# First expert layer: the subtraction that makes the next weights' low parts goes from GpSimd to VectorE, and the picks, prefix sums and places move into the middle of a tile

## The chip, the core and the metric

The kernel runs on one core of a Trainium2 chip. The metric is the device time of one execution in microseconds (us). Before the change it was 1570.85 us, the median of 3 runs (1567.33 to 1571.03).

## The reference

Three stages follow each other on 9984 rows of 256 numbers: a squared-ReLU attention without softmax over 4 batches of 2496 rows, then two mixture-of-experts layers with 8 experts each, hidden width 1024. The first layer only treats rows whose skip score is positive and adds its result to the row; the second treats all rows, with a bias on the gate by modality, and replaces the row.

```python
scores = (1.0 / S) * z @ z.T;  x = u * (relu(scores) ** 2 @ v)
# layer 1, for rows with x @ w_skip > 0
e = argmax(x @ w_gate);  g = softmax(x @ w_gate)[e]
x = x + g * (relu(x @ w1[e]) @ w2[e])
# layer 2, for all rows
logits = x @ w_gate2 + modality_bias[modality_id]
e = argmax(logits);  g = softmax(logits)[e]
out = g * (relu(x @ w1b[e]) @ w2b[e])
```

## The kernel before, in words

All products are made in single precision from two parts: a value is split into a rounded high part and a low part (value minus high), and three matmuls (high x high, high x low, low x high) are summed in PSUM.

The attention stage writes every row, with its gate and logits, to a table in device memory (`token_rows`), sorted by expert. Each expert layer (`ph` 0, then 1) is a loop over the experts, and inside it a hardware loop over tiles of 256 rows (`for t in lo..hi`, bounds read from the device's own counts). Every engine has its own instruction stream with the same loops, and semaphores join them; nothing but the order of the text sets the order within an engine. `t == lo` is the first tile of an expert.

One tile on TensorE (PE): `layer1(p)` for p = 0 to 3 makes the hidden columns (12 matmuls each, into pO), `layer2(p)` multiplies them with w2 (12 matmuls each, into pS), in the order layer1(0), layer1(1), the transposes of the next tile's rows (L1378), layer1(2), layer2(0), layer1(3), layer2(1), layer2(2), layer2(3). `layer2(p)` waits for VectorE's low part of hidden quarter p (`h_low(p)`, L1159), which waits for ScalarE's high part (`h_high(p)`, L785), which waits for layer1(p). `layer2(0)` also waits until VectorE has read the last tile's result out of pS (`y_out`; the instructions L1179 to L1186, called "the y group" below).

In the first layer a tile's result rows need routing for the second layer, one tile later: `pick_expert` on VectorE (L1109 to L1118: argmax and one-hot), `exp_tile` on ScalarE (L755), `prefix_x2` on PE (L1403 to L1405: how many rows stand ahead of each), `stage_rows` on ScalarE (L751: copy of the rows for the scatter; it waits until the last scatter has landed), `place_tile` on VectorE (L1130 to L1140: destination of each row), and two indirect DMAs from GpSimd (POOL; L579: the scatter).

The next expert's weights are in `raw` while an expert is at work. ScalarE casts them to the high parts in 4 pieces of 1024 columns (`split_high`, L633), spread over the first tile of an expert. POOL subtracts them for the low parts (`split_low`, L466, 8 instructions of 512 columns), then issues the load of the weights after those (L453, L454: 2 MB). POOL also loads w2 transposed (L458), from which PE makes gate columns at the start of an expert (L1360).

Between the layers VectorE routes the last tile, counts (`finish_groups`, up to L1073) and only then can PE enter the second layer; PE fills that time with matmuls that keep it warm (L1214).

Of the kernel before, what the change touches and what calls it, by code (L numbers as in the profile page):

```python
# [5 lines left out]
F32 = mybir.dt.float32  # L6
# [4 lines left out]
ALU = mybir.AluOpType  # L11
# [7 lines left out]
E, F = 8, 1024  # L19
# [20 lines left out]
WP = 4  # L40
# [15 lines left out]
def bass_attention_two_moe(nc, u, v, z, w_skip, w_gate, w1, w2, modality, w_gate2, bias2, w2t, out):  # L56
    xs = nc.dram_tensor("token_rows", (GR * CAP + SPARE, ROW), F32, kind="Internal").ap()

    with ExitStack() as ctx:
# [359 lines left out]
        def _(pool):  # L419
# [59 lines left out]
            def next_weights(turn_, slot):  # L479

                split_low(turn_ + 1, 1 - slot)
                e = pool.value_load(order[0:1, turn_ + 2:turn_ + 3], min_val=0, max_val=2 * E - 1)
                wait(wl_ready, WP * turn_ + 2 * WP)
                load_weights(e)
# [65 lines left out]
            for ph in range(2):  # L550
# [6 lines left out]
                for at in range(E):  # L557
# [3 lines left out]
                    def ahead():  # L561
                        if ph == 0:
                            if at + 2 < E:
                                wait(gcols_made, at + 2)
                                load_w2t(at + 2)
                            next_weights(turn_, at % 2)
                        else:
                            with pool.If(hi < total):
                                next_weights(turn_, at % 2)

                    with pool.If(lo < hi):
                        with pool.Fori(lo, hi) as t:
                            with pool.If(t == lo):
                                ahead()
# [6 lines left out]
                            else:  # L581
# [15 lines left out]
        def _(act):  # L597
# [130 lines left out]
            for ph in range(2):  # L728
# [31 lines left out]
                for at in range(E):  # L760
# [19 lines left out]
                    with act.If(lo < hi):  # L780
                        with act.Fori(lo, hi) as t:
                            def h_high(p):
                                act.wait_ge(q.h_psum, 4 * t + p + 1)
                                act.wait_ge(q.h_used, 4 * t + p + 1)
                                s_.activation(hH[p], pO[:, p * 512:(p + 1) * 512], ACT.Relu).then_inc(q.h_hi, 1)  # L785
                            def start(piece):
                                with act.If(t == lo):
                                    ahead((piece,))

                            h_high(0)  # L790
                            start(0)
                            h_high(1)
                            take_x(t + 1, (t + 1) % 2)
                            h_high(2)
                            keep_x(t + 1, (t + 1) % 2)
                            start(1)
                            if ph == 0:
                                with act.If(t > 0):
                                    exp_tile(t)
                            h_high(3)  # L800
                            start(2)
                            if ph == 0:
                                with act.If(t > 0):
                                    stage_rows(t)
                            start(3)
# [13 lines left out]
        def _(dve):  # L819
# [265 lines left out]
            for ph in range(2):  # L1085
# [55 lines left out]

                xt_low(0, 0)
# [4 lines left out]
                for at in range(E):  # L1147
                    hi = end_of(dve, ph, at)
                    if ph == 0:
# [5 lines left out]
                    with dve.If(lo < hi):  # L1155
                        with dve.Fori(lo, hi) as t:
# [4 lines left out]
                            h_low(0)  # L1161
                            h_low(1)
                            xt_low(t + 1, (t + 1) % 2)
                            h_low(2)
                            if ph == 0:
                                with dve.If(t > 0):
                                    pick_expert(t)
                            h_low(3)
                            par = t % 2
# [20 lines left out]
                            if ph == 0:  # L1190
                                with dve.If(t > 0):
                                    place_tile(t)
# [10 lines left out]
        def _(pe):  # L1203
# [186 lines left out]
            for ph in range(2):  # L1390
# [17 lines left out]
                for at in range(E):  # L1408
# [6 lines left out]
                    with pe.If(lo < hi):  # L1415
                        pe.wait_ge(wl_ready, WP * (at + 1 + ph * E))
                        pe.sem_inc(pe_passed, 1)
                        with pe.Fori(lo, hi) as t:
# [41 lines left out]
                            layer2(0)  # L1460
                            layer1(3)
# [3 lines left out]
                            last_tile(prefix_x2)  # L1465
# [33 lines left out]
```

## Time and profile before

| | |
|---|---|
| median of 3 runs | 1570.85 us |
| profiled execution | 1574.07 us, span 1572.3 us |
| PE busy | 1514.6 us (96%) |
| VectorE (DVE) busy | 1013.3 us (64%) |
| ScalarE (ACT) busy | 776.4 us (49%) |
| POOL busy | 466.1 us (30%) |
| mean granted TensorE clock | 0.988 |

Times in the rows are from the span's start. The attention stage fills about the first 740 us, the first expert layer about 750 to 1068 us, the second about 1083 to 1570 us. A PE that is busy 96% of the span still leaves some 58 us idle, and where those lie is what the rows further down show. A row's bracket gives the idle time of that engine just before the instruction, and who ended it.

### The profile page before, as it was taken

How to read it: one execution, taken by the hardware profiler on the slowest of the kernel's cores; microseconds unless marked ns; L12 is line 12 of the kernel's file. 1: busy time of each engine (PE TensorE's matmuls, PEld its weight loads, DVE VectorE, ACT ScalarE, POOL GpSimd, SP SyncE). 2: the span in 40 equal slices, each digit the busy share in tenths (PEclk: the TensorE clock that was granted, in tenths of full speed). 3: DMA queues.
4: the chain of work that ended last, by engine and by line, in shares of the span. 5: the costliest groups of instructions: out<-in, count | busy, mean ns of one | idle time of the engine just before them, and what ended most of it. 6: DMA issues, size and time to landing. Idle time of an engine off the chain costs nothing.

```text
span 1572.3 us, 38375 instructions
## 1 busy us (share of the span) xinstructions
PE 1514.6 (96%) x13409; PEld 1379.5 (88%) x13409; DVE 1013.3 (64%) x2382; ACT 776.4 (49%) x1463; POOL 466.1 (30%) x434
## 2 busy tenths in 40 slices
PE   8999999999999999998999999998999999999996
PEld 6878887788778887887988988988999999999996
DVE  7989977888788989876566666654333333333332
ACT  6677766676677767663444434443322322322321
POOL 4133412343133324222444444443211111111111
PEclk9999999999999999999999999998999999999998
DMA  5311031203002022112433333321311111111110
GB/s 114 95 42 49 27 109 33 63 31 99 27 29 62 27 82 80 30 40 92 139 126 114 127 129 126 99 79 46 101 48 41 48 54 41 48 48 41 48 48 26
DMA packets 60108, 106.41 MB, mean 68 GB/s; under 512 B 18183, under 2 KB 32018, under 8 KB 59980
## 3 DMA queue, kind: packets, MB, share of 16 engines
q1 hardware_dynamic: 41788, 46.66, 10.8%
q0 software_dynamic: 18192, 58.13, 10.8%
q8 instruction: 70, 1.15, 0.3%
q14 instruction: 58, 0.48, 0.1%
HBM read 75.35 MB, written 30.94 MB: 68 GB/s over the span
## 4 chain that ended last, share of the span: by engine, by line
PE 78%; DMA 6%; DVE 4%; issue 4%; POOL 3%; ACT 2%; POOLq 0%; DVEq 0%; SPq 0%; ACTq 0%
PE pO L1238 29%; PE pO L1430 18%; PE pS L1446 18%; PE pS L1227 8%; DMA token_rows<-xrow,dest 4%; POOL VL L466 2%; DMA raw<-in_v_dram 2%; PE pT L1378 1%; PE pT L1286 1%; DVE take L1110 1%; DMA A<-in_w2t_dram 1%; PE pO L1247 1%; DVE take L1109 1%; PE pM L1296 1%; PE pO L1360 1%
## 5 line engine op out<-in xcount | busy, mean ns | idle before, releaser
L1430 PE MATMUL pO<-ZH,VH 128*128 x2016 | 402.5, 288 | 2.3 <-issue 2.3
L1446 PE MATMUL pS<-VL,AH 128*128 128x256 f32 (+1 forms) x2016 | 370.3, 284 | 21.5 <-DVE AL L1159 21.5
L785 ACT ACTIVATE AH<-pO 128x512 fp32r<-128x512 f32 x252 | 151.0, 599 | 401.7 <-PE pO L1430 401.4
L1446 PEld LDWEIGHTS pS<-VL,AH 128*128 128x128 f32 x2016 | 311.8, 190 | 25.3 <-DVE AL L1159 25.2
L1430 PEld LDWEIGHTS pO<-ZH,VH 128*128 128x128 f32 x2016 | 328.3, 192 | 4.0 <-issue 4.0
L961 DVE TENSOR_TENSOR AL<-A,AH 128x512 fp32r<-128x512 f32 (+1 forms) x400 | 305.1, 763 | 13.7
L1238 PE MATMUL pO<-AH,VH 64*128 64x512 f32 (+1 forms) x1520 | 301.0, 386 | 3.7 <-DVE xT L870 2.3
L1238 PE MATMUL pO<-AH,VL 64*128 64x512 f32 (+1 forms) x1520 | 298.7, 383 | 0.0
L1238 PE MATMUL pO<-AL,VH 64*128 64x512 f32 (+1 forms) x1520 | 298.3, 382 | 0.0
L1159 DVE SCALAR_TENSOR_TENSOR AL<-pO,AH 128x512 fp32r<-128x512 f32 x252 | 172.7, 691 | 187.9 <-ACT AH L785 184.1
L659 ACT ACTIVATE R<-pS 128x512 f32<-128x512 f32 (+1 forms) x400 | 213.6, 587 | 157.5 <-PE pS L1227 148.4
L1430 PE MATMUL pO<-ZL,VH 128*128 x1008 | 286.0, 284 | 0.0
L1446 PE MATMUL pS<-VL,AL 128*128 128x256 f32 (+1 forms) x1008 | 284.6, 282 | 0.0
L959 DVE CAST AH<-A 128x512 fp32r<-128x512 f32 (+1 forms) x400 | 231.2, 578 | 44.6 <-ACT A L668 43.3
L668 ACT ACTIVATE A<-R 128x512 f32<-128x512 f32 (+1 forms) x400 | 228.1, 624 | 9.5 <-DVE AL L961 9.5
L1430 PEld LDWEIGHTS pO<-ZL,VH 128*128 128x128 f32 x1008 | 193.9, 192 | 0.0
L584 POOL DMA_INDIRECT out_dram<-xrow,tok_at x80 | 77.8, 973 | 382.9 <-DVE tok_at L1188 370.4
L1446 PEld LDWEIGHTS pS<-VL,AL 128*128 128x128 f32 x1008 | 190.8, 189 | 0.0
L1238 PEld LDWEIGHTS pO<-AH,VH 64*128 64x128 f32 x1520 | 147.8, 185 | 28.4 <-issue 3.4
L1238 PEld LDWEIGHTS pO<-AL,VH 64*128 64x128 f32 x1520 | 148.0, 185 | 23.2
L1238 PEld LDWEIGHTS pO<-AH,VL 64*128 64x128 f32 x1520 | 147.8, 185 | 22.3
L515 POOL TENSOR_TENSOR xT<-xT,uT 128x512 f32<-128x512 f32 x38 | 50.7, 1344 | 294.7 <-DVE xT L870 294.7
(194 smaller groups left out, 1584.4 us busy)
## 6 DMA issues: line engine op xcount, KB each, us to landing
raw<-in_w_dram POOLq DMA_DIRECT2D x22, 1024.0 KB, 7.1
xin<-token_rows SPq DMA_DIRECT2D x65, 268.0 KB
uT<-in_u_dram SPq DMA_DIRECT2D x16, 512.0 KB
A<-in_w2t_dram POOLq DMA_DIRECT2D x8, 1024.0 KB
raw<-in_v_dram SPq DMA_DIRECT2D x4, 1152.0 KB, 5.9
raw<-in_v_dram SPq DMA_DIRECT2D x4, 768.0 KB, 7.6
raw<-in_z_dram SPq DMA_DIRECT2D x8, 368.0 KB
token_rows<-pad_row SPq DMA_DIRECT2D x10, 268.0 KB
```

The costliest lines, as they stand in the source:

```text
L515: g_.tensor_tensor(xT[:, d, :], xT[:, d, :], uT[:, d, :], ALU.mult).then_inc(x_ready, 1)
L584: g_.indirect_dma_start(out, bass.IndirectOffsetOnAxis(tok_at[:, s_:s_ + 1], 0), x2a[:, s_, 0:D], None, bounds_check=N - 1, oob_is_err=Fal ...
L659: s_.activation(R[k % 2][:, 0:n], pS[k % 2][:, 0:n], ACT.Relu, scale=1.0 / S).then_inc(relu_done, 1)
L668: s_.activation(A[k % NA][:, 0:n], R[k % 2][:, 0:n], ACT.Square).then_inc(square_done, 1)
L785: s_.activation(hH[p], pO[:, p * 512:(p + 1) * 512], ACT.Relu).then_inc(q.h_hi, 1)
L959: v_.tensor_copy(AH[k % NBUF][:, 0:n], A[k % NA][:, 0:n]).then_inc(ah_ready, 1)
L961: v_.tensor_tensor(AL[k % NBUF][:, 0:n], A[k % NA][:, 0:n], AH[k % NBUF][:, 0:n].bitcast(F32), ALU.subtract).then_inc(al_ready, 1)
L1159: v_.scalar_tensor_tensor(out=hL[p], in0=pO[:, p * 512:(p + 1) * 512], scalar=0.0, in1=hH[p].bitcast(F32), op0=ALU.max, op1=ALU.subtract). ...
L1227: last = t_.matmul(pS[r][:, 0:n], w[rows, (2 * p + r) * P:(2 * p + r + 1) * P], x[rows, zc:zc + n], start=(m == 0), stop=(m == 2))
L1238: last = t_.matmul(pO[:, (KD * r + d) * QW:(KD * r + d) * QW + n], vv[rows, vo + k * D + d * P:vo + k * D + (d + 1) * P], a[k % NBUF][rows ...
L1430: last = t_.matmul(pO[:, p * 512 + fi * TT:p * 512 + (fi + 1) * TT], w[h][:, kd, f * P:(f + 1) * P], x[:, ds(par, 1), kd, :].rearrange("p ...
L1446: last = t_.matmul(pS[s][:, 0:width], a[p][:, fi * TT + s * P:fi * TT + (s + 1) * P], w[h][:, f, 0:width], start=(f == 0 and n == 0), stop ...
```

## The change

In the first layer only:

- VectorE makes the low parts of the next weights: `next_low`, 4 instructions of 1024 columns after `h_low(3)` of an expert's first tile, ahead of the y group. POOL makes none there any more. In the second layer and in the attention stage POOL still does.
- `pick_expert` moves from behind `h_low(2)` to behind `h_low(0)`; `place_tile` from behind the y group to behind `h_low(2)`.
- On PE the prefix sums move from the end of the tile to behind `layer2(0)`.
- On POOL the scatter of a tile stands ahead of the weight loads.

In both layers ScalarE's 4 casts stand together behind `h_high(3)`; in the first, `exp_tile` and `stage_rows` now stand around `h_high(2)`, ahead of `keep_x`, the copy of the next tile's rows.

```diff
-            def next_weights(turn_, slot):
-                split_low(turn_ + 1, 1 - slot)
+            def next_weights(turn_, slot, split):
+                if split:
+                    split_low(turn_ + 1, 1 - slot)
...
-                            with pool.If(t == lo):
-                                ahead()
                             if ph == 0:
                                 with pool.If(t > 0):
                                     wait(q.dest, t)
...
+                            with pool.If(t == lo):
+                                ahead()
...
                             h_high(0)
-                            start(0)
                             h_high(1)
                             take_x(t + 1, (t + 1) % 2)
-                            h_high(2)
-                            keep_x(t + 1, (t + 1) % 2)
-                            start(1)
                             if ph == 0:
                                 with act.If(t > 0):
                                     exp_tile(t)
+                                    h_high(2)
+                                    stage_rows(t)
...
+                            keep_x(t + 1, (t + 1) % 2)
                             h_high(3)
-                            start(2)
...
+                            with act.If(t == lo):
+                                ahead(range(WP))
...
+                def next_low(turn_, slot):
+                    for n, (raw, wh, wl) in enumerate(weight_pieces(slot)):
+                        dve.wait_ge(wh_ready, WP * turn_ + n + 1)
+                        v_.tensor_tensor(wl, raw, wh.bitcast(F32), ALU.subtract).then_inc(wl_ready, 1)
...
                             h_low(0)
+                            if ph == 0:
+                                with dve.If(t > 0):
+                                    pick_expert(t)
                             h_low(1)
                             xt_low(t + 1, (t + 1) % 2)
                             h_low(2)
                             if ph == 0:
                                 with dve.If(t > 0):
-                                    pick_expert(t)
+                                    place_tile(t)
                             h_low(3)
+                            if ph == 0:
+                                with dve.If(t == lo):
+                                    next_low(turn_ + 1, 1 - at % 2)
...
-                            if ph == 0:
-                                with dve.If(t > 0):
-                                    place_tile(t)
...
                             layer2(0)
+                            last_tile(prefix_x2)
                             layer1(3)
                             layer2(1)
                             layer2(2)
                             layer2(3)
-                            last_tile(prefix_x2)
```

VectorE before, in a tile of the first layer, from the end of the pick on: `AL<-pO,AH` is `h_low(3)`, and `xrow<-pS,xkeep` opens the y group.

```order
L1118 TENSOR_TENSOR oh<-eq,take 128x2x8
L1166 UNCONDITIONAL_BRANCH
L1158 REGISTER_ALU
L1159 SCALAR_TENSOR_TENSOR AL<-pO,AH 128x512
L1170 REGISTER_ALU
L1179 ISA
L1179 REGISTER_ALU
L1179 SCALAR_TENSOR_TENSOR xrow<-pS,xkeep 128x256
```

VectorE now, at the same place: `dest<-dest_f,take` ends the place, and the two rows at L1143 are the four subtractions, run only where `t == lo`.

```order
L1137 TENSOR_TENSOR dest<-dest_f,take 128x2
L1173 UNCONDITIONAL_BRANCH
L1162 REGISTER_ALU
L1163 SCALAR_TENSOR_TENSOR AL<-pO,AH 128x512
L1177 COMPARE_AND_BRANCH
L1143 TENSOR_TENSOR VH<-raw,VH 128x1024 x2
L1143 TENSOR_TENSOR VL<-raw,VL 128x4x256 x2
L1177 UNCONDITIONAL_BRANCH
L1180 REGISTER_ALU
L1189 ISA
L1189 REGISTER_ALU
L1189 SCALAR_TENSOR_TENSOR xrow<-pS,xkeep 128x256
```

So between `h_low(3)` and the y group there are now four subtractions, and the place has gone from behind the y group to a point ahead of `h_low(3)`.

ScalarE before, from `h_high(2)` on: `xkeep<-xin` is `keep_x`, the casts from `raw` stand one by one.

```order
L785 ACTIVATE AH<-pO 128x512
L739 ISA
L739 COPY xkeep<-xin 128x536
L787 COMPARE_AND_BRANCH
L633 CAST VH<-raw 128x1024
L787 UNCONDITIONAL_BRANCH
L798 COMPARE_AND_BRANCH
L755 ACTIVATE ex<-lsh 128x2x8
L798 UNCONDITIONAL_BRANCH
L783 REGISTER_ALU
L785 ACTIVATE AH<-pO 128x512
```

ScalarE now, from `h_high(2)` on, with `stage_rows` (`xrow<-xrow`) between it and `keep_x`.

```order
L786 ACTIVATE AH<-pO 128x512
L751 ISA
L752 COPY xrow<-xrow 128x536
L791 UNCONDITIONAL_BRANCH
L784 REGISTER_ALU
L786 ACTIVATE AH<-pO 128x512
L795 UNCONDITIONAL_BRANCH
L740 ISA
L740 COPY xkeep<-xin 128x536
L784 REGISTER_ALU
L786 ACTIVATE AH<-pO 128x512
```

The copy for the scatter has come ahead of the last quarter's high part, and no cast stands between the quarters any more.

## Rows read from the trace of the kernel before

**Rows 1.** Stages: engines' busy us (x instructions), granted clock, DMA share, GB/s.

```profile
750.00:1069.00 319.00, 297.49 (x2585) 290.24 (x2585) 196.07 (x610) 131.34 (x235) 140.61 (x128) 0.99 0.35 115
1069.00:1084.00 15.00, 9.34 (x103) 8.88 (x101) 7.74 (x44) 1.88 (x4) 3.88 (x4) 0.75 0.14 46
1084.00:1572.00 488.00, 474.42 (x3999) 474.21 (x3998) 176.45 (x360) 143.34 (x244) 89.64 (x90) 0.99 0.16 49
```

**Rows 2.** PE's wait between 750 and 1069 us: us, times, longest.

```profile
PE pS L1446 <- DVE AL L1159: 21.5, 18, 2.7
```

**Rows 3.** Timeline of PE: start, us; transposes of four tiles.

```profile
765.46 0.38 PE L1378 MATMUL pT<-ident,xin 128*128 128x128 f32 x2
...
777.63 0.27 PE L1378 MATMUL pT<-ident,xin 128*128 128x128 f32 x1
...
791.17 0.38 PE L1378 MATMUL pT<-ident,xin 128*128 128x128 f32 x2
...
1057.26 0.38 PE L1378 MATMUL pT<-ident,xin 128*128 128x128 f32 x2
```

**Rows 4.** Timeline of the third expert's three tiles, 829 to 871 us.

```profile
835.90 5.04 POOL L466 TENSOR_TENSOR VH<-raw,VH 128x512 fp32r<-128x512 f32 x4
...
837.28 3.70 DVE L1110 TENSOR_SCALAR take<-take 128x2 f32<-128x2 f32 x1
...
850.31 0.51 PE L1446 MATMUL pS<-VL,AH 128*128 128x264 f32 x2 [0.69 <-DVE AL L1159]
...
852.44 1.02 POOL L579 DMA_INDIRECT token_rows<-xrow,dest  x1 [0.30 <-issue]
...
859.36 0.64 ACT L751 COPY xrow<-xrow 128x536 f32<-128x536 f32 x1 [4.88 <-DMA token_rows<-xrow,dest]
...
863.80 0.39 PE L1446 MATMUL pS<-VL,AH 128*128 128x264 f32 x1 [0.99 <-DVE AL L1159]
```

**Rows 5.** Stages again: a stretch with a lower granted clock.

```profile
910.00:920.00 10.00, 7.29 (x49) 6.97 (x49) 6.77 (x16) 3.16 (x5) 8.08 (x8) 0.83 0.42 150
```

**Rows 6.** Timeline of an undisturbed tile of the first layer.

```profile
768.78 0.16 DVE L1109 TENSOR_SCALAR take<-xrow 128x2 f32<-128x2 f32 x1
...
770.30 0.17 DVE L1118 TENSOR_TENSOR oh<-eq,take 128x16 bf16<-128x16 f32 x1
...
770.41 0.60 ACT L785 ACTIVATE AH<-pO 128x512 fp32r<-128x512 f32 x1 [0.60 <-PE pO L1430]
...
775.06 0.49 DVE L1179 SCALAR_TENSOR_TENSOR xrow<-pS,xkeep 128x256 f32<-128x256 f32 x1 [3.33 <-PE pS L1446]
...
776.12 0.17 DVE L1186 COPY xrow<-xkeep 128x6 f32 x1
...
779.50 0.41 PE L1446 MATMUL pS<-VL,AH 128*128 128x264 f32 x2
```

**Rows 7.** VectorE's subtraction in the attention stage (ns), and one beside a scatter.

```profile
L961 DVE TENSOR_TENSOR AL<-A,AH x400: 624/693/1709, 10.7 to 725.0; 128x512 fp32r<-128x512 f32 x107, 128x448 fp32r<-128x448 f32 x27
...
674.31 0.74 DVE L961 TENSOR_TENSOR AL<-A,AH 128x512 fp32r<-128x512 f32 x1
674.32 0.97 POOL L496 DMA_INDIRECT token_rows<-xrow,dest  x1 [0.30 <-issue]
```

**Rows 8.** POOL's weight loads, and ScalarE's cast.

```profile
L633 ACT CAST VH<-raw 128x1024 fp32r<-128x1024 f32 x16 | 16.8, 1048 | 0.0
...
849.88 0.92 POOL L454 DMA_DIRECT2D raw<-in_w_dram  x1
```

**Rows 9.** Timeline between the two layers.

```profile
1075.10 6.01 PE L1214 MATMUL pS<-ones 128*128 128x128 bf16 x64
1077.59 0.64 ACT L751 COPY xrow<-xrow 128x536 f32<-128x536 f32 x1 [4.70 <-DMA token_rows<-xrow,dest]
...
1081.75 0.17 DVE L1073 CAST pad_from<-base_t 128x8 int32<-128x8 f32 x1
...
1083.39 0.57 PE L1430 MATMUL pO<-ZH,VH 128*128 x1 [2.28 <-issue]
```

More of the change, by code:

```diff
@@ L565, in ahead @@
                                 load_w2t(at + 2)
-                            next_weights(turn_, at % 2)
+                            next_weights(turn_, at % 2, False)
                         else:
                             with pool.If(hi < total):
-                                next_weights(turn_, at % 2)
+                                next_weights(turn_, at % 2, True)
                     with pool.If(lo < hi):
                         with pool.Fori(lo, hi) as t:
-                            with pool.If(t == lo):
-                                ahead()
                             if ph == 0:
@@ L580, in _ @@
                                                               bounds_check=GR * CAP - 1, oob_is_err=False).then_inc(q.stored, 16)
-                            else:
+                            with pool.If(t == lo):
+                                ahead()
+                            if ph == 1:
                                 wait(q.y2_out, t + 1)
@@ L785, in h_high @@
                                 s_.activation(hH[p], pO[:, p * 512:(p + 1) * 512], ACT.Relu).then_inc(q.h_hi, 1)
-                            def start(piece):
-                                with act.If(t == lo):
-                                    ahead((piece,))
                             h_high(0)
-                            start(0)
                             h_high(1)
                             take_x(t + 1, (t + 1) % 2)
-                            h_high(2)
-                            keep_x(t + 1, (t + 1) % 2)
-                            start(1)
                             if ph == 0:
@@ L799, in _ @@
                                     exp_tile(t)
-                            h_high(3)
-                            start(2)
-                            if ph == 0:
-                                with act.If(t > 0):
-                                    stage_rows(t)
-                            start(3)
+                                    h_high(2)
+                                    stage_rows(t)
+                                with act.Else():
+                                    h_high(2)
+                            else:
+                                h_high(2)
+                            keep_x(t + 1, (t + 1) % 2)
+                            h_high(3)
+                            with act.If(t == lo):
+                                ahead(range(WP))
                     with act.Else():
@@ L1148, in _ @@
                     hi = end_of(dve, ph, at)
+                    turn_ = at + ph * E
                     if ph == 0:
@@ L1189, in _ @@
                                 v_.memset(mx[:, 0:1, 0:1], 0.0).then_inc(q.y_out, 1)
-                            if ph == 0:
-                                with dve.If(t > 0):
-                                    place_tile(t)
+                    if ph == 0:
+                        with dve.Else():
+                            next_low(turn_ + 1, 1 - at % 2)
                     lo = hi
```

## The prediction, made before the changed kernel was run

> **What bounds the kernel now.** I read the stages first, then the waits of the one that the change touches, then its timeline. In the stages [rows 1] the reader sees that PE is busy 297.5 of 319 us in the first expert layer, 9.3 of 15 us between the layers, and 474 of 488 us in the second layer. So what PE waits for is what can be won, and it lies mostly in the first layer. In its waits [rows 2] one pair holds PE: layer2 waits for VectorE's low part of a hidden quarter, 18 times, 21.5 us. VectorE itself is idle a third of that stage (196 of 319 us busy), so it isn't out of throughput; it is late at certain places.
>
> How much that costs in all is read from the distance of the tiles [rows 3]. Two undisturbed tiles are 777.63 - 765.46 = 12.17 us apart; with a change of expert between them (gate columns) it is 791.17 - 777.63 = 13.54 us. From 765.46 to the last tile at 1057.26 there are 21 steps, 7 of them changes of expert: 14 x 12.17 + 7 x 13.54 = 265.2 us, and the trace takes 291.8. That is 26.6 us too much, and with the wait of about 1.5 us in the last tile, which lies behind 1057.26, 28 us. 21.5 of them are the waits; 2 x 1.7 are two drops of the granted clock from 2.4 to 1.2 GHz, of which the rows show one [rows 5] (10 x 0.17), both beside long waits of PE (it is busy only 7.3 of 10 us there); the rest hides in the modelled ends of the matmuls.
>
> The timeline of one expert [rows 4] shows three causes. (a) In the first tile a two-column TENSOR_SCALAR of the pick takes 3.70 us: it starts at 837.28 and ends at 840.98, within 0.04 us of the end of POOL's four subtractions (835.90 + 5.04). Undisturbed, the same group runs from 768.78 to 770.47 as a whole [rows 6]. `h_low(3)` stands behind it, and so does layer2. (b) In the second tile the y group and the place stand ahead of `h_low(0)`: PE waits 0.69 us. (c) POOL, held up by subtractions and loads, issues its scatter at 852.44 only, ScalarE's `stage_rows` waits 4.88 us for it to land, the y group waits for that copy, and `h_low(0)` is late again: 0.99 us.
>
> **The change part by part.** POOL's 8 subtractions per expert go, and with them (a) whole: nothing else of POOL's runs long enough to hold VectorE for 3 us. The scatter now goes ahead of the loads, so (c) goes: a scatter that is issued in mid tile has about a tile, 12.17 us, until `stage_rows` of the next tile asks for it, and even behind weight loads it needed 859.36 - 852.44 = 6.9 us. The place leaves the stretch between the y group and `h_low(0)`, and (b) goes: without it `h_low(0)` can start when ScalarE has the high part. All of the 28 us is therefore open.
>
> Here a rule of the Trainium skill bears on (a). SBUF — State Buffer, section "Who interferes with whom", says that whoever issues first gets the port pair that VectorE and GpSimd share for its whole instruction. By it the small instruction would wait for the end of one GpSimd instruction, 5.04 / 4 = 1.26 us, where the trace shows 3.70 us, the end of the run of four. By the rule removing (a) would be worth less than half of what it is by the row; the sum goes by the row.
>
> What is added is 4 subtractions of 1024 columns on VectorE. The trace has none of that width. From below: 693 ns for 512 columns, 624 ns for 448 [rows 7], so 69 ns for 64 columns and 0.69 + 8 x 0.069 = 1.25 us for 1024. From above: twice 0.69 = 1.39 us undisturbed, and twice 1.71 = 3.4 us if each ran at the longest that this instruction ever took. I take 1.25: a single instruction has its fixed part once. ScalarE's casts at 1.05 us [rows 8] are faster and don't pace it.
>
> Where it lies, counted from `h_high(3)` of an expert's first tile as zero (770.41 in the clean tile [rows 6]): the first cast is ready at 0.5 + 1.05 = 1.6, the subtractions end at 1.6 + 4 x 1.25 = 6.6. The y group, so far at 775.06 (4.65), comes at 6.6 + 0.35 (register steps) and takes 776.12 + 0.17 - 775.06 = 1.23: it ends at 8.15, and `h_low(0)` at 8.85. PE asks for it at 779.50, which is 9.1. So it is hidden with 0.25 us to spare. A group of 12 matmuls takes (9.09 - 0.5) / 6 = 1.43 us, since six of them and the transposes (0.5 us) lie in those 9.09 us. Behind `h_low(0)` the pick takes 1.6 us beyond its start, to about 10.4, and PE's prefix sums now ask for it at 9.1 + 1.43 = 10.5; the place (1.5 us), `h_low(1)` to `h_low(3)` and the next rows' low part (0.6 us from one start to the next) take 1.5 + 4 x 0.6 more, to about 14.4, where layer2(3) asks at 10.6 + 3 x 1.43 = 14.9. Every step fits with little to spare, in the tile behind the first one of each expert. The cover is thin, and one thing eats it: the y group ends with a small copy, and the pick begins with small TENSOR_SCALARs, just when POOL issues the two weight loads (0.76 and 0.92 us [rows 8]), and rows show that such instructions can be held by POOL. Bounds for the new wait: 0 and 1.68 - 0.25 = 1.4 us per expert. I take 0.6, for 8 experts 5 us (0 to 11).
>
> The new waits on one engine: on ScalarE `exp_tile` stands ahead of `h_high(2)`, and behind it queue `h_high(2)`, `stage_rows`, `keep_x` and `h_high(3)`. The pick's part that it waits for ends 0.8 us after `h_low(0)`, at 9.6 in the worst tile, when layer1(2) has only just ended (9.1); layer2(2) asks at 13.5. Nothing. The later `keep_x` delays the load of the next rows by about 2 us of a slack that no wait in [rows 2] has ever used. The load of w2 transposed comes some 7 us later in the expert and is wanted at the next one's start, over 12 us on; every expert here has 2 or 3 tiles. In the second layer ScalarE's casts stand in one block of 4.2 us behind `h_high(3)`, and the next `h_high(0)` comes four groups of PE, 5.7 us, after it: hidden. I cost these at nothing.
>
> Between the layers [rows 9]: `stage_rows` of the last tile waits 4.70 us for a scatter that was issued late, because the place stood behind the y group; and the whole routing of the last tile hangs on it, up to the counts at 1081.75, and PE enters at 1083.39. With the place in mid tile that scatter has landed, and the pick comes about 1.2 us earlier: the counts come 5.5 us earlier, at 1076.2. But PE's 64 warming matmuls take 6.01 us and end at 1081.1 today. They start when the prefix sums have ended, 1.2 us earlier, so they end at 1079.9 and PE can enter 1.5 us later: at 1081.4. The granted clock of this stretch is 0.75 on average [rows 1]; at the full clock throughout they would take some 2 us less, and PE would enter at about 1079.2. So the gain is 2.0 to 4.2 us, with 0 and 5.5 as outer bounds; I take 3.
>
> Sum: -28 + 5 - 3 = -26 us. The profiled execution, 1574.07 us (span 1572.3, 1.8 us around it), would be 1548; it lies 3.2 us above the median of the runs, so on that scale 1570.85 - 26 = 1544.8 us.
>
> **The rivals.** First, the gain is halved by a wait that takes the place of the removed one: the four subtractions meet POOL's scatter of the same tile. For it speaks the narrow cover above: every us on them is a us on PE. If each of the two scatter DMAs (0.97 us) held them, the y group would come 1.9 us later, less 0.25, and with the same again in part for the prefix sums some 2 us per expert: 8 x 2 = 16 instead of 5 us, 1570.85 - 28 + 16 - 3 = 1556 us. Against it: in the attention stage the same instruction met a scatter alone 57 times, the first at 93.34 us and the last at 674.31, and took 0.69 to 0.76 us [rows 7]. The skill's same section speaks for it: a VectorE instruction with two SBUF inputs contends with a GpSimd instruction that reads SBUF, as the scatter reads its indices; by that rule the 57 should have been held, and the trace does not agree.
>
> Second, slower than before: VectorE becomes the bound of the tile behind each expert's first. Its place is the four subtractions, its price their length. They cost PE nothing up to 1.25 us, and the gain of 31 us is used up when each takes 1.25 + (31 / 8 + 0.25) / 4 = 2.3 us. At 3.4 us, the upper bound, the loss would be 8 x (4 x 2.15 - 0.25) = 67 us and the time 1570.85 - 31 + 67 = 1607 us. For it: this instruction did take 1.71 us at 512 columns. Against it: that was beside subtractions or products of POOL, and in the first layer POOL has none of these left.
>
> Third, no change: PE's waits only move, because the real limit of the late tiles is the landing of the scatter, and that is no faster. It would have to be over 12 us on the way; 6.9 us is the most seen here. 1571 us.
>
> **How the numbers follow.** The forecast, with its own range of 1538 (28 + 4.2 won, nothing lost) to 1552, has 0.67; the halved gain 0.21; slower 0.06; no change 0.03; a gain above all bounds, by the clock, 0.03. The predicted time is the forecast's, 1544.8 us. The range goes from 1538 to 1558 and leaves out the last three cases and the tail of the second. A difference of 0.3% (4.7 us) is about what a measurement of this kernel can tell from no change. Faster: 0.67 + 0.21 + 0.03 = 0.91; within 0.3%: 0.03; slower: 0.06.
>
> **What would show it.** Right: the small instructions of the pick all at 0.2 to 0.5 us; no wait of `stage_rows` for the scatter; four subtractions near 1.25 us per expert; tiles 12.2 us apart within an expert; PE's waits for `h_low` under 6 us in the layer; the second layer 11.8 us per tile as before; PE entering it right behind the warming matmuls. Wrong: subtractions over 2 us; PE waiting for the one-hot or for `h_low(0)` in every second tile by over 1 us; waits of PE for rows or weights that it never had; a second layer whose tiles have grown.

## The result, and the profile after

The changed kernel took 1543.69 us (median of 4 runs, 1540.86 to 1543.97) beside 1570.18 us for the kernel before on the same chip: 0.983 of the time, 95% interval 0.981 to 0.985. Measured again on another occasion (run 9 below) it was 1544.12 us and 0.983 (0.982 to 0.985). The prediction said 1544.8. The number was right, and, as the rows below show, partly because errors of opposite sign met.

The stages of the profiled execution (1540.86 us, span 1539.2), columns as in [rows 1]:

```profile
750.00:1045.00 295.00, 293.19 (x2667) 289.40 (x2665) 201.19 (x683) 130.65 (x238) 70.28 (x68) 1.00 0.38 125
...
1054.00:1539.00 485.00, 467.00 (x3932) 466.59 (x3930) 173.28 (x356) 139.80 (x239) 89.67 (x90) 0.98 0.16 48
```

In the first layer PE is now busy all but 1.8 us. Its waits from 744 to 1100 us, all but one of 0.7 and one of 0.5 us, as in [rows 2]:

```profile
PE pS L1456 <- DVE AL L1163: 3.2, 1, 3.2
PE pO L1380 <- DVE pad_from L1070: 2.9, 1, 2.9
PE pM L1413 <- DVE oh L1115: 1.6, 1, 1.6
...
```

The 18 waits for low parts (21.5 us) are gone. The one that is left, 3.2 us, isn't in the first layer at all: it ends at 1077.50, in the third tile of the second. The transposes of PE, the answer to [rows 3]:

```profile
762.71 0.60 PE L1388 MATMUL pT<-ident,xin 128*128 128x128 f32 x4
774.89 0.60 PE L1388 MATMUL pT<-ident,xin 128*128 128x128 f32 x4
788.48 0.60 PE L1388 MATMUL pT<-ident,xin 128*128 128x128 f32 x4
1027.06 0.60 PE L1388 MATMUL pT<-ident,xin 128*128 128x128 f32 x4
```

12.18 us from tile to tile and 13.59 with a change of expert; the 21 steps take 1027.06 - 762.71 = 264.35 us, where they took 291.8 and an undisturbed run of them was put at 265.2. (That was about 1 us too high: at the last change of expert there are no gate columns to make, and that step takes at most 12.4 us.)

The VectorE subtractions, and the small TENSOR_SCALAR that was held for 3.70 us in [rows 4] (ns, minimum, median, maximum). "Held" means here: much longer than the same instruction is undisturbed, and at its end together with an instruction of GpSimd.

```profile
L1143 DVE TENSOR_TENSOR VH<-raw,VH x16: 1219/1222/1226, 757.2 to 1010.5; 128x1024 fp32r<-128x1024 f32 x16
```
```profile
L1107 DVE TENSOR_SCALAR take<-take x23: 168/169/657, 763.7 to 1038.8; 128x2 f32<-128x2 f32 x23
```

One turn of the weights in the third expert, with the tile behind it, in which everything was to fit narrowly:

```profile
831.53 0.60 ACT L786 ACTIVATE AH<-pO 128x512 fp32r<-128x512 f32 x1 [1.39 <-PE pO L1440]
...
833.10 2.36 DVE L1143 TENSOR_TENSOR VH<-raw,VH 128x1024 fp32r<-128x1024 f32 x2 [0.24 <-ACT VH L634]
...
833.46 1.70 POOL L578 DMA_INDIRECT token_rows<-xrow,dest  x1 [0.30 <-issue]
...
835.38 2.36 DVE L1143 TENSOR_TENSOR VL<-raw,VL 128x1024 fp32r<-128x1024 f32 x2
...
838.70 0.16 DVE L1196 COPY xrow<-xkeep 128x6 f32 x1
838.77 0.68 DVE L1163 SCALAR_TENSOR_TENSOR AL<-pO,AH 128x512 fp32r<-128x512 f32 x1
...
839.23 0.91 POOL L454 DMA_DIRECT2D raw<-in_w_dram  x1
...
839.56 0.57 DVE L1107 TENSOR_SCALAR take<-take 128x2 f32<-128x2 f32 x1
...
840.45 0.41 PE L1456 MATMUL pS<-VL,AH 128*128 128x264 f32 x2
...
841.29 0.17 DVE L1115 TENSOR_TENSOR oh<-eq,take 128x16 bf16<-128x16 f32 x1
...
841.90 0.18 PE L1413 MATMUL pM<-oh,before 128*128 128x16 bf16 x1
```

Counted from `h_high(3)` at 831.53, rounded: the subtractions end at 6.2 (predicted 6.6), the y group at 7.3 (8.15), `h_low(0)` at 7.9 (8.85), PE asks at 8.9 (9.1); the one-hot is there at 9.9 (10.4) and asked for at 10.4 (10.5). The cover, the time from a value being ready to PE asking for it, is 1.0 us and 0.4 us, where 0.25 and 0.1 were predicted. The 0.57 us of the TENSOR_SCALAR, 0.17 undisturbed, lie beside a weight load of GpSimd (839.23 + 0.91 = 840.14, the TENSOR_SCALAR ends at 840.13); 0.66 is the longest of it.

Between the layers, the answer to [rows 9]:

```profile
1040.37 0.18 PE L1413 MATMUL pM<-oh,before 128*128 128x16 bf16 x1 [1.60 <-DVE oh L1115]
...
1041.19 3.74 PE L1224 MATMUL pS<-ones 128*128 128x128 bf16 x64
...
1045.63 0.38 PE L1440 MATMUL pO<-ZH,VH 128*128 x1 [0.71 <-DVE ZL L1093]
```

The 64 warming matmuls take 3.74 us instead of 6.01: the granted clock was 1.00 from 1041.2 to 1045.6, where it was 0.60 from 1075.1 to 1081.1 before. What differs just ahead of them is PE's wait for the one-hot between the layers, 1.60 us now and 3.07 before; behind the 3.07 us the clock had fallen to 0.50. Waits further back don't explain it: run 4 below has waits of up to 5.4 us in its first layer and 1.39 here, and its warming takes 3.74 us; run 3 has hardly any in the first layer and 3.3 us here, and takes 4.59. Run 7 doesn't fit so simply, with 1.61 us here and 5.36 us of warming; its first layer has eight waits of 1.2 us. What decides there stays open.

The start of the second layer is new:

```profile
1060.28 5.07 POOL L466 TENSOR_TENSOR VL<-raw,VL 128x512 fp32r<-128x512 f32 x4
...
1066.13 0.77 POOL L453 DMA_DIRECT2D raw<-in_w_dram  x1 [0.78 <-POOL VL L466]
...
1069.48 1.02 POOL L585 DMA_INDIRECT out_dram<-xrow,tok_at  x1 [0.30 <-issue]
...
1075.90 0.88 DVE L1194 TENSOR_SCALAR xrow<-pS,xkeep 128x256 f32<-128x256 f32 x2 [9.21 <-DMA out_dram<-xrow,tok_at]
...
1076.76 0.68 DVE L1163 SCALAR_TENSOR_TENSOR AL<-pO,AH 128x512 fp32r<-128x512 f32 x1
...
1077.50 0.80 PE L1456 MATMUL pS<-VL,AH 128*128 128x256 f32 x2 [3.20 <-DVE AL L1163]
```
```profile
1060.43 0.60 PE L1388 MATMUL pT<-ident,xin 128*128 128x128 f32 x4
...
1072.27 0.60 PE L1388 MATMUL pT<-ident,xin 128*128 128x128 f32 x4
...
1088.83 0.60 PE L1388 MATMUL pT<-ident,xin 128*128 128x128 f32 x4
```
```profile
1070.00:1074.00 4.00, 4.00 (x36) 4.00 (x35) 0.00 (x0) 1.75 (x3) 0.51 (x1) 1.00 1.03 339
1074.00:1078.00 4.00, 0.80 (x5) 0.60 (x4) 2.10 (x7) 1.24 (x2) 0.26 (x1) 0.87 0.23 84
1078.00:1082.00 4.00, 4.00 (x27) 4.00 (x27) 1.24 (x3) 0.07 (x1) 1.68 (x2) 0.70 0.46 134
```

Read the first block from the bottom: PE waits in the third tile for `h_low(0)`, which stands on VectorE behind the second tile's y group; that waits until the first tile's result rows have left their buffer. The DMA that takes them is issued at 1069.48, behind the subtractions and both weight loads, and 2 MB of weights fill the DMA engines ahead of it (share 1.03, 339 GB/s). VectorE goes on 6.4 us after its issue. PE's wait is 3.2 us, and the clock falls behind it. The two stretches behind 1074 lose 4 x 0.13 + 4 x 0.30 = 1.7 us by it, of which 3.2 x 0.08 = 0.3 us lie in the wait itself (granted clock 0.92 from 1074.3 to 1077.5) and cost nothing: about 1.5 us more. The tile steps say the same: 11.84 us from transposes to transposes, and 16.56 here, 4.7 more. It happens once, since the second layer has a single set of subtractions and weight loads, in its first tile.

So by stage, in the two profiles: from the first expert's gate columns (746.36 before, 744.35 after) to the first warming matmul (1068.20 and 1036.36; 40 of them stand ahead of the 64 above) 321.8 us before and 292.0 after (-29.8); from there to the first matmul of the second layer 15.2 and 9.3 (-5.9); the second layer 488.9 and 493.6 (+4.7). What lies ahead of the first layer differs by 2.0 us with no edit in it; over all the profiled executions, before and below, it varied from 742.9 to 746.4.

### The profile page after: what moved, and what is told of

It reads as the page before. It is cut to its first block, busy times and chain, and to the rows that moved or that the text cites. A ratio compares the mean times of both kernels' runs of the same rounds, so it can differ in the third digit from the quotient of the medians.

```text
span 1539.2 us, 38120 instructions
## 1 busy us (share of the span) xinstructions
PE 1501.9 (98%) x13409; PEld 1369.7 (89%) x13409; DVE 1010.4 (66%) x2414; ACT 773.9 (50%) x1463; POOL 391.2 (25%) x370
## 3 DMA queue, kind: packets, MB, share of 16 engines
q8 instruction: 70, 1.15, 0.3%
## 4 chain that ended last, share of the span: by engine, by line
PE 91%; DMA 3%; issue 2%; POOL 1%; DVE 1%; ACT 1%; SPq 0%; DVEq 0%; POOLq 0%; ACTq 0%
PE pO L1248 31%; PE pO L1440 23%; PE pS L1456 23%; PE pS L1237 9%; PE pT L1388 2%; DMA raw<-in_v_dram 2%; PE pT L1296 1%; DMA A<-in_w2t_dram 1%; PE pO L1257 1%; PE pM L1306 1%; PE pO L1370 1%; POOL VL L504 0%; DMA out_dram<-xrow,tok_at 0%; ACT R L660 0%; POOL VL L466 0%
```

## The experiments

Ten runs, in the order in which they were taken. "Layer 1", "between" and "layer 2" are the three stretches just named. The kernel before was run beside each, median 1569.5 to 1570.2 us. Runs 1, 2, 9 and 10 are medians of 5 executions, 5 and 8 of 10, the others of 4.

| run | what | median us | ratio, 95% | layer 1 | between | layer 2 |
|---|---|---|---|---|---|---|
| | before | 1570.2 | 1 | 321.8 | 15.2 | 488.9 |
| | changed | 1543.7 | 0.983 (0.981 to 0.985) | 292.0 | 9.3 | 493.6 |
| 1 | casts spread in layer 2 | 1537.5 | 0.979 (0.977 to 0.981) | 292.9 | 9.3 | 489.8 |
| 2 | rows written first in layer 2 | 1537.3 | 0.980 (0.978 to 0.982) | 291.9 | 9.3 | 489.8 |
| 3 | subtraction alone | 1543.7 | 0.984 (0.981 to 0.986) | 295.0 | 13.5 | 490.0 |
| 4 | moves alone | 1588.6 | 1.012 (1.010 to 1.014) | 339.9 | 9.1 | 492.0 |
| 5 | before, GpSimd pieces halved | 1577.8 | 1.004 (1.002 to 1.006) | 328.5 | 15.0 | 490.6 |
| 6 | one subtraction more | 1548.5 | 0.986 (0.984 to 0.988) | 298.3 | 9.3 | 493.4 |
| 7 | two more | 1558.8 | 0.992 (0.990 to 0.994) | 307.3 | 10.6 | 494.1 |
| 8 | before, one-element TENSOR_SCALARs | 1567.1 | 0.998 (0.997 to 0.999) | 320.1 | 13.3 | 487.4 |
| 9 | changed, again | 1544.1 | 0.983 (0.982 to 0.985) | 292.0 | 9.3 | 494.1 |
| 10 | edits of 1 and 2 | 1537.7 | 0.979 (0.978 to 0.980) | 292.5 | 9.3 | 489.7 |

**Runs 1, 2, 9 and 10: the second layer.** Run 1 gives the second layer its spread casts back, on ScalarE:

```diff
                             h_high(0)
+                            start(0)          # ph == 1, t == lo: ahead((0,))
...
                             keep_x(t + 1, (t + 1) % 2)
+                            start(1)
                             h_high(3)
-                            with act.If(t == lo):
-                                ahead(range(WP))
+                            if ph == 0:
+                                with act.If(t == lo):
+                                    ahead(range(WP))
+                            start(2)
+                            start(3)
```

> The changed kernel, with ScalarE's four casts of the second layer at their old places in the tile (behind the first, third and fourth quarter), the first layer untouched. The changed kernel's trace has one wait of 3.20 us of PE in the second layer and a drop of the granted clock behind it, in the tile after the first; before there was none. Theory: the casts in one block behind the fourth quarter start POOL's subtractions some 6 us later, these and the weight loads hold up POOL's scatter of the finished rows, the tile's result group on VectorE waits for the scatter's landing, and layer2(0) with it. Then this kernel has no such wait and takes 3.2 + 1.7 = about 5 us less than the changed one, some 1539 us. Rival: the wait comes from something else that the second layer inherited (the earlier entry, the load of rows), then it stays and the time is 1544 us.

Run 2 moves the loads on GpSimd instead, and leaves the casts in a block:

```diff
-                            with pool.If(t == lo):
-                                ahead()
+                            if ph == 0:
+                                with pool.If(t == lo):
+                                    ahead()
                             if ph == 1:
                                 wait(q.y2_out, t + 1)
...
+                                with pool.If(t == lo):
+                                    ahead()
```

> The changed kernel, with POOL's scatter ahead of the subtractions and weight loads in the second layer too, as the change does it in the first; the casts stay in one block. Theory: it is the scatter's place behind the subtractions that makes VectorE's result group wait in the second tile; with the scatter first the wait of 3.20 us goes and the time is about 1539 us, as with the casts spread. Rival: the subtractions themselves hold VectorE in that tile wherever the scatter stands; then PE still waits 2 to 4 us for a low part and the time stays at 1544 us.

Both took the wait away, and 6 us. (PE's wait lies in the layer's third tile, one later than run 1's expectation says.) In run 2 the rows leave before the subtractions:

```profile
1060.31 0.97 POOL L586 DMA_INDIRECT out_dram<-xrow,tok_at  x1 [15.39 <-DVE tok_at L1201]
...
1062.58 5.06 POOL L466 TENSOR_TENSOR VH<-raw,VH 128x512 fp32r<-128x512 f32 x4
```

In run 1 GpSimd subtracts early instead, and its weight loads, and the rows behind them, come sooner: 15.7 us after the layer's first matmul (1047.16) and not 20.5 (1066.13 - 1045.63):

```profile
1062.85 0.77 POOL L453 DMA_DIRECT2D raw<-in_w_dram  x1 [0.78 <-POOL VL L466]
```

VectorE still sits idle until the rows have landed in both runs, 4.9 and 5.0 us, as in the kernel before (5.0); in the changed kernel it was 9.2 us, and only that reached PE.

Runs 9 and 10 put the changed kernel and both edits together side by side.

> The changed kernel as it is, five rounds, beside the next run. Theory (the second layer's first tile costs it 4 to 5 us, and runs 1 and 2 each took that away): 1543 to 1544 us again, and over 4 us more than the next run. Rival (the 6 us between the changed kernel and runs 1 and 2 lay in the chip or in the hour, since they were measured on another occasion): 1537 to 1540 us, level with the next run.

> The changed kernel with both edits of runs 1 and 2: in the second layer the casts are spread over the first tile as in the kernel before, and GpSimd writes a tile's result rows before it subtracts and loads. Theory (each edit alone removes the same wait): 1537 us, as each alone, since there is nothing left for the second edit to remove; no wait of TensorE for VectorE in the second layer. Rival (each removed a part of it): 1534 to 1535 us.

1544.12 (1541.92 to 1544.86) against 1537.70 us (1536.54 to 1538.77): the ranges and the intervals are apart, so the 6 us are the kernel's and not the occasion's, and the second edit has nothing left to remove. In run 9's profile the wait is there again, 3.4 us. By the profiles the second layer is 3.8 to 4.4 us shorter; the other 2 us lie in executions that were not profiled (the profiled one was the changed kernel's fastest both times), and stay open. Each of the kernels of runs 1, 2 and 10 beats both the changed one and the one before.

**Run 3: the subtraction alone.** The four subtractions stay on VectorE; picks, prefix sums, places, scatter, casts and `stage_rows` go back to where they were.

```diff
+                            h_high(2)
+                            keep_x(t + 1, (t + 1) % 2)
+                            start(1)
...
                             h_low(0)
-                            if ph == 0:
-                                with dve.If(t > 0):
-                                    pick_expert(t)
                             h_low(1)
...
-                                    place_tile(t)
+                                    pick_expert(t)
...
+                                with dve.If(t > 0):
+                                    place_tile(t)
```

> The kernel before with only the subtraction moved: VectorE makes the four low parts of the first layer behind the fourth quarter of an expert's first tile; picks, prefix sums, places, casts and scatters stay where they were. Theory: the hold of 3.7 us goes (PE 1.8 us per expert), but the place still stands between the result group and the next first quarter and now begins some 2 us later, so PE waits 1 to 2 us there, and the scatter still lands late. Net 1 us per expert: about 1561 us, a third of the gain. Rival: POOL's subtractions were the whole cause, so this alone brings the time to about 1545 us.

The rival was right: layer 1 falls from 321.8 to 295.0 us, 27 of the 30 us, with every move undone. Its waits of PE, and ScalarE's wait for the late scatter:

```profile
PE pM L1417 <- DVE oh L1119: 3.3, 1, 3.3
...
PE pS L1460 <- DVE AL L1167: 1.4, 4, 0.6
```
```profile
ACT xrow L752 <- DMA token_rows<-xrow,dest: 31.0, 10, 4.5
```

The one-hot's wait of 3.3 us lies between the layers. `stage_rows` still waits ten times, 31 us, and PE loses 1.4 us by it at most. The moves are worth 3.0 us in layer 1 and 4.2 between the layers, and their casts in a block lose 3.6 in layer 2; the medians, 1543.71 and 1543.69, show nothing of the difference.

**Run 4: the moves alone.** All moves stay; GpSimd subtracts.

```diff
-                            next_weights(turn_, at % 2, False)
+                            next_weights(turn_, at % 2, True)
...
-                            if ph == 0:
-                                with dve.If(t == lo):
-                                    next_low(turn_ + 1, 1 - at % 2)
```

> The changed kernel with the subtraction of the first layer back on POOL: picks, prefix sums, places, the block of casts and the scatter ahead of the loads as in the changed kernel. Theory: the casts in one block make POOL's eight subtractions one run of 10 us behind the fourth quarter, and that run now covers the small copy that ends the result group and the small TENSOR_SCALARs of the next pick; each is held to the run's end, the next first quarter comes at about 12 us where PE asks at 9.1, and PE waits some 3.5 us per expert: 1544 + 28 = about 1570 us, no gain over the kernel before. Rival: the moves were what counted and POOL's subtractions hurt only where the pick stood: then about 1548 us.

Slower than before, 1.2%, which neither theory had. With the casts in a block GpSimd's eight subtractions run without a gap, and one small copy of VectorE is held to 854.00, the end of the seventh of them:

```profile
845.26 5.05 POOL L466 TENSOR_TENSOR VH<-raw,VH 128x512 fp32r<-128x512 f32 x4
...
847.45 6.55 DVE L1193 COPY xrow<-xkeep 128x6 f32 x1
...
850.27 4.94 POOL L466 TENSOR_TENSOR VL<-raw,VL 128x512 fp32r<-128x512 f32 x4
...
854.65 0.81 PE L1450 MATMUL pS<-VL,AH 128*128 128x264 f32 x2 [3.84 <-DVE AL L1163]
```
```profile
PE pS L1450 <- DVE AL L1163: 29.1, 7, 5.4
```

PE waits 3.8 to 5.4 us in each of seven experts; the granted clock of the stretch from 750 to 1095 us is 0.94, where the changed kernel's first layer has 1.00.

**Run 5: how the hold works.** The kernel before, with GpSimd's pieces cut from 512 to 256 columns.

```diff
-                    for half in range(2):
-                        w = half_piece(n, half)
+                    for quarter in range(4):
+                        w = quarter_piece(n, quarter)
```

> The kernel before, with POOL's subtractions of both expert layers cut to 16 of 256 columns in place of 8 of 512. Theory: a small VectorE instruction in the two-port mode is held until POOL's run of subtractions ends, as the 3.70 us row shows; halving the single instruction shortens no run, so PE's waits stay (18 of them, some 21 us) and the time is 1570 us, or a few us more for POOL's fixed cost. Rival, the Trainium skill's rule (SBUF — State Buffer, Who interferes with whom): the hold lasts for one GpSimd instruction; then the holds shrink to about 0.7 us, the wait in an expert's first tile goes and the time falls by some 10 us to 1560.

In most experts many small instructions are held one after the other, mostly by 0.2 to 0.6 us each:

```profile
838.70 4.90 POOL L472 TENSOR_TENSOR VH<-raw,VH 128x256 fp32r<-128x256 f32 x7
...
840.80 0.76 DVE L1120 TENSOR_TENSOR eq<-lg,mx 128x16 f32<-128x16 f32 x1
```

and in two of them one instruction of 16 elements is held through eight of GpSimd's, here to their end at 802.36, and PE waits 6.3 and 6.6 us behind them:

```profile
796.28 6.11 DVE L1124 TENSOR_TENSOR oh<-eq,take 128x16 bf16<-128x16 f32 x1
796.87 5.49 POOL L472 TENSOR_TENSOR VL<-raw,VL 128x256 fp32r<-128x256 f32 x8
```

So neither "to the end of one GpSimd instruction" nor "to the end of the run" holds by itself. The kernel before has both kinds too: holds of 1.0 to 1.2 us that end with a single instruction of GpSimd, and one of 3.78 us (at 908.94) that ends with the third of four. Which of them an instruction meets isn't settled. Smaller pieces don't help on the whole: 0.4% slower, with executions from 1567.6 to 1581.8 us.

**Runs 6 and 7: the cover.** One and two further subtractions of 1024 columns per expert, into an unused buffer:

```diff
                         dve.wait_ge(wh_ready, WP * turn_ + n + 1)
+                        if n < 1:
+                            spare = (uT, xT)[n][:, :, :].rearrange("p k s -> p (k s)")
+                            v_.tensor_tensor(spare, raw.rearrange("p a b -> p (a b)"), wh.bitcast(F32).rearrange("p a b -> p (a b)"), ALU.subtract)
                         v_.tensor_tensor(wl, raw, wh.bitcast(F32), ALU.subtract).then_inc(wl_ready, 1)
```

That is run 6; run 7 has `if n < 2`.

> The changed kernel with one more subtraction of 1024 columns per expert (the first piece once more, into a buffer that is unused there). It measures the cover. The changed kernel's trace has 0.95 us between the first low part and layer2(0), and 0.4 us between the one-hot and the prefix sums, in the tile behind an expert's first. Theory: 1.22 us more takes both and PE waits 0.8 us per expert at the prefix sums: 8 x 0.8 = 6 us, about 1550 us. Rival: VectorE's slack there is larger than the trace's distance (something else is late too), then nothing changes: 1544 us.

> The same with two more subtractions per expert, 2.44 us. Theory: PE waits 2.0 us per expert, 16 us in all, and a drop of the granted clock or two may come with waits of this length: 1560 to 1565 us. Rival: the waits don't add up because ScalarE and POOL have slack: under 1550 us.

PE's wait for the one-hot in run 6, and the larger pair of them in run 7. One of the 8 is that of the last tile (1.6 us), one of the 9 that of the second layer (3.3 us), which both are in the changed kernel too:

```profile
PE pM L1416 <- DVE oh L1115: 3.9, 8, 1.6
```
```profile
PE pS L1459 <- DVE AL L1166: 12.7, 9, 3.3
```

PE waits 0.3 us seven times for the one-hot, and with two subtractions more 1.2 us eight times for `h_low(0)`. Layer 1 grows by 6.3 us and then by 9.0 more: 0.8 and 1.1 us per expert for 1.22 us of work each. So the real cover is 1.22 - 0.8 = 0.4 us, and behind it a us on VectorE is nearly a us on PE. The waits in the rows are smaller than the time lost: in run 6 the tile behind an expert's first takes about 12.97 us where the changed kernel's takes 12.17, and the other tiles are as they were, but the row shows 0.3 of these 0.8 us as a wait. The ends of matmuls are modelled, and here they hide the rest; lengths of tiles and stages tell more.

**Run 8: which instructions are held.** The kernel before, with the two-column TENSOR_SCALARs of the pick and the place cut into instructions of one column.

```diff
-                    step(v_.tensor_scalar(take[:, 0:T, 0], x2a[:, :, TOK], float(N), None, ALU.is_lt))
+                    v_.tensor_scalar(take[:, 0:1, 0], x2a[:, 0:1, TOK], float(N), None, ALU.is_lt)
+                    step(v_.tensor_scalar(take[:, 1:2, 0], x2a[:, 1:2, TOK], float(N), None, ALU.is_lt))
```

```profile
832.98 5.07 POOL L466 TENSOR_TENSOR VH<-raw,VH 128x512 fp32r<-128x512 f32 x4
...
834.24 0.15 DVE L1111 TENSOR_SCALAR take<-take 128x1 f32<-128x1 f32 x1
...
834.70 3.40 DVE L1115 TENSOR_TENSOR lsh<-lg,mx 128x16 f32<-128x16 f32 x1
```

834.70 + 3.40 = 838.10, where GpSimd ends at 838.05.

## Why the number was right, and which steps were not

- **The 28 us in layer 1 and their removal: right**, 27.4 us between the transposes of [rows 3] and of after, 29.8 us by the stage (1.6 more in the last tile, 0.7 ahead of the first of these transposes).
- **The subtraction at 1.25 us, not held by the scatter: right.** 1.22 us, 32 times, at most 1.226. The first rival fell with it. It was GpSimd's scatter that was held instead: 1.70 us beside the subtraction (1.64 to 1.98 in the eight experts), where it takes 0.97 alone, and nobody waited for it.
- **Cause (a): right in kind and too small in share.** The prediction gave it one of three places, and explained (b) by the y group and the place standing ahead of `h_low(0)`. Run 3 puts them back there and PE still loses only 1.4 us in waits. What was overlooked is that in (b), too, small instructions were held by GpSimd's second run of subtractions; these rows are of the kernel before, same expert as [rows 4]:

```profile
843.28 5.07 POOL L466 TENSOR_TENSOR VL<-raw,VL 128x512 fp32r<-128x512 f32 x4 [2.33 <-ACT VL L633]
...
846.08 1.03 DVE L1186 COPY xrow<-xkeep 128x6 f32 x1
...
847.22 1.15 DVE L1131 TENSOR_SCALAR den<-den 128x2 f32<-128x2 f32 x1
```

  Both take 0.17 us undisturbed: 1.8 us lost, where PE waited 0.69. The page's rule that the prediction weighed (SBUF — State Buffer, "Who interferes with whom", in the Trainium skill: the pair is held for one whole instruction) would give (a) 1.26 us, and the row of 3.70 us doesn't agree; with the two rows here, 1.03 and 1.15 us, it would. Run 3's 27 us don't decide between them, since they hold (a) and (b) together. Cause (c) is the same kind: with no subtractions on GpSimd the late scatter still costs ScalarE 31 us (40.5 before) and PE next to nothing.
- **The new wait, 5 us: mis-sized; it was none.** Every position was put late: 0.35 us of register steps between the subtractions and the y group don't exist, and the subtractions ended 0.4 us earlier. The weight loads' hold, bounded at 1.68 us, was 0.66 - 0.17 = 0.5 us at most, on one instruction of the pick, and the copy was never held. The cover that decides is 0.4 us (run 6), not 0.1; the mechanism is as described, and run 7 shows it at work.
- **Between the layers, 3 us: mis-sized; it was 5.9**, above even the outer bound of 5.5. By the rows the wait for the one-hot is 1.5 us shorter, the transposes behind it 0.6, the warming matmuls 2.3, and the gap ahead of the second layer's first matmul 1.6. The prediction named the full clock as a case (entry 2 us sooner) and did not take it as the likeliest.
- **The second layer "hidden": failed.** The step looked at ScalarE only, whose `h_high(0)` indeed never waits for the block of casts. It did not follow the casts to GpSimd: subtractions that start late end late, behind them stand the weight loads and only then the DMAs of the result rows, and the y group of the next tile waits for these. +4.7 us in the profile, all of it in one tile of 16.56 us (tiles that have grown stand among the prediction's own signs of being wrong); about 6 in the medians by runs 1, 2 and 10. In layer 1 the same order had been changed (scatter ahead of the loads), in layer 2 not.

The terms: -29.8 instead of -28 + 5 = -23, -5.9 instead of -3, and +4.7 instead of 0: -31.0 against -26 by the profiles. The medians differ by 26.5 only; the profiled execution of before was 3.9 us above its median, that of after 2.8 below, and 2.0 us of the 33.2 between them lie ahead of layer 1. Where the remaining 4.7 us sit in a usual execution is open. Against the medians the error in layer 2 is what made the sum come out right: without it the time would have been 1537.5 us, just below the prediction's own range.

## What to carry to other kernels

Before crediting a move, look at every small instruction in the stretch for one that is longer than its own median, and at what GpSimd runs beside it: here one shared cause stood behind three waits that looked different, and taking GpSimd's subtractions away gave the whole gain (27 of 30 us in the first layer, and the same median), while the moves without it cost 18 us. A block of work that is moved later on one engine must be followed through every engine that it feeds, to the last DMA in that queue, and the buffer which that DMA sets free. And a term for a clock that fell behind a wait goes with the wait.

## What the runs showed of the hardware that was not expected

- A VectorE instruction of 2 to 16 columns can be held through several back-to-back GpSimd TENSOR_TENSORs: 3.70 us and 3.40 (a run of four at 1.27 us each), 6.55 (out of eight), 6.11 (eight of 0.7). The longest in the kernel before is 4.49. Run 5 shows short holds, mostly 0.2 to 0.6 us extra and so within one of GpSimd's instructions, and two long ones in the same trace. Short or long, they have one thing in common: of the small VectorE instructions between 744 and 1110 us of six traces (before, after, runs 3, 4, 5 and 8), some 150 took at least 0.09 us more than their median, and every one of these ended within 0.1 us of the end of an instruction of GpSimd.
- One-column TENSOR_SCALARs and TENSOR_REDUCEs were never held (0.14 to 0.17 us in run 8); two-column TENSOR_SCALARs, a 128x6 copy and a TENSOR_TENSOR with two inputs of 16 elements were. Nor was `h_low`, which reads one of its operands out of PSUM: 0.68 to 0.69 us in the kernel before, all 252 times, 11 of them beside GpSimd's subtractions in the first layer.
- Between the large subtraction and a GpSimd indirect DMA it is the DMA instruction that loses: 1.70 us, at most 1.98, beside VectorE subtractions of 1.22 us that didn't grow. A two-column TENSOR_SCALAR loses against the same DMA: 0.46 us instead of 0.17 in the kernel before (781.14 + 0.46 = 781.60, where the DMA instruction ends too), and 0.57 to 0.66 beside a weight load.
